# Right sides of a block-triangular solve, moved between its steps, and work for the next pair moved into an MLP stage

## The reference

```python
y[t] = r[t] @ state
Sa = state @ a[t]
state = state * w[t][None, :] - outer(Sa, b[t]) + outer(v[t], k[t])
```

## Time and profile before

| | us |
|---|---|
| median of 3 runs | 1704.86 |
| all runs | 1708.75, 1697.19, 1704.86 |
| the profiled execution | 1699.7 |
| its span in the profile | 1697.9 |
| mean granted clock of TensorE over it | 0.943 |

### The profile page before, as it was taken

One profiled execution on the slowest core, in us unless ns is written; L12 is line 12 of the kernel. 1 busy time (PEld: TensorE's weight loads), 2 busy tenths in 40 slices (PEclk: granted clock), 3 DMA queues, 4 the chain that ended last, 5 costly groups with the idle time before them and its releaser, 6 DMA issues. The chain is left out here.

```text
span 1697.9 us, 37853 instructions
## 1 busy us (share of the span) xinstructions
PE 1495.4 (88%) x15888; PEld 1296.8 (76%) x15888; DVE 801.4 (47%) x1395; ACT 423.2 (25%) x859; POOL 375.8 (22%) x314
## 2 busy tenths in 40 slices
PE   1298476998998998998996779999999999999998
PEld 0266355976876887797786769999999999999998
DVE  6866844956855765493311143333333333333332
ACT  0032233333333333333332221111111111111111
POOL 4121354323323333131232350202020201010000
PEclk9988677999998997999998989999999999999999
DMA  6534475056046126203001041000001010100011
GB/s 186 145 102 130 121 198 155 5 150 176 17 112 184 47 54 166 74 1 108 19 1 35 20 159 34 15 19 7 27 0 34 0 34 0 34 0 0 0 46 46
DMA packets 89410, 112.83 MB, mean 66 GB/s; under 512 B 10952, under 2 KB 67400, under 8 KB 89288
## 3 DMA queue, kind: packets, MB, share of 16 engines
q1 hardware_dynamic: 89288, 111.05, 23.3%
HBM read 78.73 MB, written 32.28 MB: 65 GB/s over the span
## 5 line engine op out<-in xcount | busy, mean ns | idle before, releaser
L1332 PE MATMUL banks<-x2t,u 128*128 x1536 | 377.3, 393 | 9.2 <-POOL u L1299 9.2
L1342 PE MATMUL banks<-u,hid 128*128 128x320 f32 x2304 | 360.6, 309 | 0.0
L1342 PEld LDWEIGHTS banks<-u,hid 128*128 128x128 f32 x2304 | 349.0, 188 | 11.2
L1332 PEld LDWEIGHTS banks<-x2t,u 128*128 128x128 f32 x1536 | 284.0, 189 | 62.2 <-issue 9.5
L1397 DVE SCALAR_TENSOR_TENSOR hid<-banks,hid 128x512 fp32r<-128x512 f32 x192 | 132.8, 692 | 414.5 <-ACT hid L1367 414.5
L1367 ACT ACTIVATE hid<-banks 128x512 fp32r<-128x512 f32 x192 | 115.0, 599 | 582.0 <-PE banks L1332 582.0
L769 PE MATMUL banks<-xt,wi 128*128 128x512 f32 x768 | 197.2, 400 | 19.6 <-issue 12.4
L778 PE MATMUL banks<-wo,hid 128*128 128x320 f32 x1152 | 183.8, 309 | 5.7 <-POOL hid L1169 5.7
L778 PEld LDWEIGHTS banks<-wo,hid 128*128 128x128 f32 x1152 | 175.3, 188 | 14.1 <-POOL hid L1169 6.4
L769 PEld LDWEIGHTS banks<-xt,wi 128*128 128x128 f32 x768 | 142.5, 191 | 47.5 <-issue 20.8
L1169 POOL TENSOR_TENSOR hid<-gap,hid 128x512 fp32r<-128x512 f32 x96 | 123.7, 1288 | 225.3 <-ACT hid L909 225.0
(11 more groups left out here) (105 smaller groups left out, 1558.3 us busy)
## 6 DMA issues: line engine op xcount, KB each, us to landing
scaled_operands<-made SPq DMA_DIRECT2D x42, 416.8 KB
made<-kbaw SPq DMA_DIRECT2D x42, 312.0 KB
kb<-scaled_operands SPq DMA_DIRECT2D x24, 416.0 KB
raw<-w SPq DMA_DIRECT2D x8, 640.0 KB, 5.7
lam<-scaled_operands SPq DMA_DIRECT2D x24, 209.6 KB
at<-scaled_operands SPq DMA_DIRECT2D x24, 208.0 KB
raw<-w SPq DMA_DIRECT2D x8, 512.0 KB, 4.0
rt<-rvt SPq DMA_DIRECT2D x96, 40.0 KB
```

The source lines that it names most:

```text
L1332: mm = pe.matmul(p_up[f][:], u1[:, par, w, f * 128:(f + 1) * 128], xt[:, x, cols], start=(i == 0), stop=(i == 7))
L1342: mm = pe.matmul(p_dn[t][:, 0:D], hid[:, f, h, t * 128:(t + 1) * 128], u2[:, par, w, f, :], start=(f == 0 and i == 0), stop=(f == NFU - 1 ...
```

## The change

`right_sides` takes a block b and makes only that. Block 0 stays at the head of the pair; blocks 1 to 3 go in front of the rest of their own step (block 1 in front of `turn_state`), each behind a wait for VectorE's copy of the block before. `sma_full` is raised for block 0 by the right sides, as before by all of them. `scores_low` comes ahead of `turn_answers` on PE, and their copies change places on ScalarE.

`load_kb_a` is split. `load_a` now stands in front of `load_v`, behind the decays, and waits for all four blocks of the pair's own right sides.

For the pair behind an MLP, SyncE issues the loads of v (natural), kb, r, the decays and the raw units, and the late store, in the MLP, ahead of its wait for the stage's output. The two diagonals that PE made in that pair (24 and 25, 32 and 33, 40 and 41) are made in the MLP behind the fourth `up`, into the bank of the turned answers, and ScalarE copies them in front of the output. A wait in `turn_state` keeps that bank until they are copied.

```diff
--- before.py
+++ after.py
@@ -223,17 +223,26 @@
         result_bank = pairs[3][:, 1, :]
         STATE = slice(C, C + 2 * GH // 2 * HD)
 
-        def diagonal_bank(i):
-
-            return result_bank if i < FIRST and i % 2 else state_bank
+        def drained(p):
+
+            return p % PPC == PPC - 1 and p >= PPC
+
+        def in_mlp(p):
+
+            return prepared_in(p) if p >= 0 and drained(p) else []
+
+        late_diagonals = [i for p in range(NP) for i in in_mlp(p)]
+
+        def diagonal_of(i):
+
+            if i in late_diagonals:
+                k = late_diagonals.index(i) % 2
+                return turn_bank[:, k * C:(k + 1) * C]
+            return (result_bank if i < FIRST and i % 2 else state_bank)[:, 0:C]
 
         def answer_rows(j, b):
 
             return block_of((b + 2 * j) % NB)
-
-        def drained(p):
-
-            return p % PPC == PPC - 1 and p >= PPC
 
         down_bank = [pairs[1][:, 0, :], pairs[1][:, 1, :], answer_bank, state_bank]
 
@@ -339,7 +348,7 @@
                     sp.wait_ge(op_stored[slot(i)], 16 * uses(i))
                 return scratch[2 * p:2 * p + 2, :, :].rearrange("j p w -> p j w")
 
-            def load_kb_a(p):
+            def load_kb(p):
 
                 both = both_units(p)
                 if p >= 2:
@@ -347,9 +356,13 @@
                     sp.wait_ge(low_full, p - 1)
                 sp.dma_start(kb[:, p % 2, :, :, :, :].rearrange("p j a q t -> p j (a q t)"), both[:, :, 0:OP_A])\
                     .then_inc(kb_in[p % 2], 16)
+
+            def load_a(p):
+
+                both = both_units(p)
                 if p >= 2:
                     for j in range(2):
-                        sp.wait_ge(sma_full[j], NB * (p - 2) + 1)
+                        sp.wait_ge(sma_full[j], NB * (p - 1))
                 a = at[:, p % 2, :, :, :].rearrange("p j q t -> p j (q t)")
                 sp.dma_start(a, both[:, :, OP_A:OP_LAM]).then_inc(at_in[p % 2], 16)
 
@@ -436,11 +449,13 @@
                 for i in range(FIRST):
                     store_operands(i)
                     if i == 2:
-                        load_kb_a(0)
+                        load_kb(0)
+                        load_a(0)
                         load_decays(0)
                     if i == 5:
                         load_r(1)
-                        load_kb_a(1)
+                        load_kb(1)
+                        load_a(1)
                     if 0 < i <= 8:
                         load_raw(i - 1 + RING)
 
@@ -449,34 +464,42 @@
                 for i in prepared_in(p)[1:]:
                     store_operands(i)
 
+            def early_loads(p):
+
+                if p + 1 < NP:
+                    load_v_natural(p + 1)
+                if p + 2 < NP:
+                    load_kb(p + 2)
+                if p:
+                    store_late(p - 1)
+
             def pair(p):
                 c = p // PPC
+                after_mlp = p > 0 and drained(p - 1)
                 raws = loaded_in(p)
                 if p == 0:
                     load_v(1)
-                if p + 1 < NP:
-                    load_v_natural(p + 1)
-                if p + 2 < NP:
-                    load_kb_a(p + 2)
-                if p and not drained(p - 1):
-                    store_late(p - 1)
-                for i in raws[:1]:
-                    load_raw(i)
-                if p + 2 < NP:
-                    load_r(p + 2)
-                for i in raws[1:]:
-                    load_raw(i)
+                if not after_mlp:
+                    early_loads(p)
+                    for i in raws[:1]:
+                        load_raw(i)
+                    if p + 2 < NP:
+                        load_r(p + 2)
+                    for i in raws[1:]:
+                        load_raw(i)
                 if p == 2 * PPC - 1:
                     load_tokens(0)
                 elif p % PPC == 0 and p >= 2 * PPC:
                     load_tokens(c - 1)
                 for i in prepared_in(p)[:1]:
                     store_operands(i)
-                if p and not drained(p - 1):
-                    store_tokens(p - 1)
-                if p + 1 < NP:
-                    load_decays(p + 1)
+                if not after_mlp:
+                    if p:
+                        store_tokens(p - 1)
+                    if p + 1 < NP:
+                        load_decays(p + 1)
                 if p + 2 < NP:
+                    load_a(p + 2)
                     load_v(p + 2)
                 if 0 <= p - PIECES_FROM < PIECES // 2:
                     raw_piece(2 * (p - PIECES_FROM))
@@ -486,8 +509,17 @@
                 if c < 0:
                     return
                 if last is not None:
-                    store_late(last)
+                    p = last + 1
+                    if p < NP:
+                        early_loads(p)
+                        if p + 2 < NP:
+                            load_r(p + 2)
                     store_tokens(last)
+                    if p < NP:
+                        if p + 1 < NP:
+                            load_decays(p + 1)
+                        for i in loaded_in(p):
+                            load_raw(i)
                 if c == NCH - 1:
                     load_tokens(c)
                 sp.wait_ge(x2_saved_v, 2 * (c + 1))
@@ -504,9 +536,11 @@
             def diagonal(i):
 
                 _, b_made, a_made, _ = parts(i)
-                o = diagonal_bank(i)
+                o = diagonal_of(i)
                 pe.wait_ge(scaled, 2 * (i + 1))
-                if i >= FIRST:
+                if i in late_diagonals:
+                    pe.wait_ge(ut_saved, (i - FIRST) // 2 + 1)
+                elif i >= FIRST:
                     pe.wait_ge(lt_saved, i)
                 elif i >= 2:
                     pe.wait_ge(lt_saved, i - 1)
@@ -516,25 +550,29 @@
                                        a_made[rows(s), q, block_of(b)], start=True, stop=True)
                 mm.then_inc(lt_full, 1)
 
-            def right_sides(p, j):
+            def right_sides(p, j, b):
 
                 g = 2 * (p % PPC) + j
                 o = solve_bank(j)
-                if j == 0:
-                    if p >= PPC:
-                        pe.wait_ge(state_ready, p - PPC + 1)
-                    pe.wait_ge(vn_in[p % 2], 16 * (p // 2 + 1))
-                    if p % PPC == 0 and p >= 2 * PPC:
-                        pe.wait_ge(up_saved, NF1 * (p // PPC - 1))
-                pe.wait_ge(sc_saved[j], p + 1)
-                for b in range(NB):
-                    t, d = block_of(b), slice(b * HD, (b + 1) * HD)
-                    for h, q, s in heads:
-                        pe.matmul(o[block_of(h), d], at[:, p % 2, j, q, t], st[:, g, q, rows(s)], start=b == 0, stop=False)
-                    for h, q, s in heads:
-                        mm = pe.matmul(o[block_of(h), d], nvmak[:, j, s, 1, q, t], vnat[:, p % 2, j, h, :],
-                                       start=False, stop=b == NB - 1)
-                mm.then_inc(sma_full[j], 1)
+                if b == 0:
+                    if j == 0:
+                        if p >= PPC:
+                            pe.wait_ge(state_ready, p - PPC + 1)
+                        pe.wait_ge(vn_in[p % 2], 16 * (p // 2 + 1))
+                        if p % PPC == 0 and p >= 2 * PPC:
+                            pe.wait_ge(up_saved, NF1 * (p // PPC - 1))
+                    pe.wait_ge(sc_saved[j], p + 1)
+                else:
+                    pe.wait_ge(rhs_saved[j], NB * p + b)
+                t, d = block_of(b), slice(b * HD, (b + 1) * HD)
+                for h, q, s in heads:
+                    pe.matmul(o[block_of(h), d], at[:, p % 2, j, q, t], st[:, g, q, rows(s)], start=b == 0, stop=False,
+                              skip_group_check=b > 0)
+                for h, q, s in heads:
+                    mm = pe.matmul(o[block_of(h), d], nvmak[:, j, s, 1, q, t], vnat[:, p % 2, j, h, :],
+                                   start=False, stop=True, skip_group_check=b > 0)
+                if b == 0:
+                    mm.then_inc(sma_full[j], 1)
 
             def right_side_rest(p, j, b):
 
@@ -561,6 +599,8 @@
 
                 if p:
                     pe.wait_ge(ut_saved, p)
+                    if in_mlp(p - 1):
+                        pe.wait_ge(lt_saved, diagonals_before(p + 1))
                 else:
                     pe.wait_ge(kbn_saved[1], 1)
                 for j in range(2):
@@ -708,11 +748,11 @@
                     diagonal(i)
 
             def pair(p):
-                prepared = prepared_in(p - 1)
                 after_mlp = p > 0 and drained(p - 1)
+                prepared = [] if after_mlp else prepared_in(p - 1)
                 more = p + 1 < NP
-                right_sides(p, 0)
-                right_sides(p, 1)
+                right_sides(p, 0, 0)
+                right_sides(p, 1, 0)
                 if after_mlp:
```

(21 more changed lines are left out.)

## The result

| | before | changed |
|---|---|---|
| median of 13 runs, us | 1704.06 | 1684.22 |
| lowest and highest | 1690.78, 1713.89 | 1675.84, 1695.09 |
| profiled execution and its span | 1699.7, 1697.9 | 1691.96, 1690.3 |

A forecast was written before the change was run, and what follows sets the result against it. It took PE's work plus 0.86 us of idle time per pair to bound the recurrence, with stalls and half clock lengthening some pairs. Terms summed to +1.6 us; between 1699.7 and the 1704.9 median bases it stated 1704, range 1683 to 1727.

The forecast's parts named there:

- the sum: All forecast terms over the recurrence and the pairs behind an MLP added up: +1.6 us on an execution of 1699.7.
- rival A: Heads of pairs: thinner heads remove three quarters of stalls and half-clock time, -20 in place of -2, 1686 us; chance 0.25.
- The undisturbed pair: Steady pair's head: blocks add 1.01 us, earlier scores of answers save 0.45, net +0.56; idle 0.2 then 1.2 us.
- The pairs behind an MLP: Pairs 8, 12, 16, 20: head and blocks +3.1 us; loads made in the MLP -6.7, between 0 and -10.
- Rival C: Behind an MLP: output and tokens cause the low clock, so moved loads gain 5.4 us less; 1709 us; chance 0.15.
- The load of a: Moved behind the decays: no cost there; leaving the burst at the head cuts stalls by 2 us, between 0 and -10.
- Rival B: Heads of pairs: new idle time lowers the clock, ten more falls in twelve heads, +21 us, 1725 us; chance 0.18.
- my test: Recurrence, 504 to 834 us: the prediction is wrong if the mean clock there moves by more than 0.05.

The follow-up runs named there:

- e1: Kernel before plus only the MLP part: loads and diagonals of the pair behind an MLP made in the MLP; 1688.6 us, ratio 0.9927.
- e3: Kernel before with only the load of a moved to its new place, in front of `load_v`; 1700.0 us, ratio 1.0000.
- e4: Changed kernel with all four blocks of right sides at the head again; 1685.4 us, ratio 0.9921 to before.
- e6: Changed kernel with one block at the head and the other three in one run behind the first answers; 1705.8 us, ratio 1.0028 to before.
- e11: The changed kernel measured again, unaltered, on the same chip as three other runs; 1687.4 us, ratio 0.9892 to before.
- e9: Changed kernel with block 0 of the right sides made twice at the head to fill idle time, output unchanged; 1682.6 us, ratio 0.9858 to before.
- e7: e4 with most rows of kb, a, r, v and v natural not loaded from pair 10's operands on, output wrong; 1666.4 us, ratio 0.9781 to before.
- e5: Changed kernel with the second block of right sides moved to the head too, two between the steps; 1663.1 us, ratio 0.9759 to before.

## Why the prediction came out as it did

The forecast of no measurable change, 1704 with 1683 to 1727, holds by its range and only just: 1684.2 is at its lower edge, and the sum of +1.6 us stands against some -16. That is luck of the range, which was drawn wide enough for rival A; the sum missed. The two profiles say where: pairs 0 to 7 came out at +4.4 us (the sum's terms for them give +4.3), the stages of pairs 8, 12, 16 and 20 at -8.7 (-3.6), and the other pairs at -4.7 (+2.9); the terms that are left, -2.0, were tied to no pair.

**The undisturbed pair: right.** L687, the former L647, starts 2.58 us behind the turned answers where it started 3.48 behind; the low scores are ahead of them now. The pair is 0.46 us longer (forecast 0.56), the idle time 1.28 us (1.4) and ended by the copy that was named. VectorE's update of the state splits it, 0.24 and 0.81, which I had not seen. A block costs 0.32 (from 513.46 to 513.78 in PE's timeline, forecast 0.34), and the MLPs with two diagonals in them are 1.0 us longer (61.36 to 62.4, forecast 0.9).

**The pairs behind an MLP: right in kind, mis-sized.** Stages 8, 12 and 16 are 9.4 us shorter together, pair 20's 0.7 longer as forecast (+0.7). With +0.8 for each of the three, the loads give -11.8 where my term was -6.7, "between 0 and -10". The clock did what was forecast, the pairs take 13.5, 13.2 and 13.7 us, and VectorE's wait of 5.34 us for a raw unit in pair 12 is gone. The reason for taking two thirds, output and tokens together at the head, had no effect: all four pairs run at 1.00. Alone the part gave 12 us (e1). Rival C is out.

**The load of a: no cost shows, as said; of the -2 nothing shows either** (e3: 0.0 us, give or take 5, with 15.5 us of late time ahead of diagonals, where it was 15.3).

**The term that the sum lacked: late instructions.** I read them as the effect of a burst of transfers, and let the spread of the right sides count for nothing there. e4 against the changed kernel shows that it removes 12 of 20 us, as much as the seven waits behind fast blocks cost before (11.7), and e6 that they come back with the run. It offsets most of the 0.9 us a pair that spreading costs. And the clock often falls with these waits: behind pair 8 of the kernel before, seven of the nine falls to the low level come within a wait with no releaser or up to 1.3 us behind it, and the other two are behind MLPs. This is rival A's result in part, through a cause that I gave only as "thins out all three". Three quarters of the stalls and of the low clock were to vanish; it was 61% of late time (20.1 to 7.8), and in pairs 9 to 23 half clock went from 61 to 44 us, or 34 in e11.

**Rival B came in part.** The new idle time took the clock in pairs 21 to 23 (+7.5 us in that profile, +2.5 in e11) and in pair 17, but not in the ten of twelve that would have made the change a loss. The rule of the Trainium skill that stands beside B (TensorE: Matmul & The Clock Gate, "A second HAM failure mode: psum-queue depth-cycling") agrees with e9 and with the 12 falls at 1.55 us; for the changed kernel as a whole the falls it foretells were too few to make a loss.

The mean clock from 504 to 834 us, my test, moved from 0.92 to 0.94, less than 0.05; it hides that the stages of pairs 14 to 19 all rose and pairs 22 and 23 fell.

## What to carry to other kernels

Work that can be put off is best placed where an engine would wait anyway, no more of it and no less: the head had 1.3 us of waiting, one block at it left a gap that cost clock, four made a run that outpaced its own instructions, and two or three were some 20 us better than either. A long run of very short matmuls has a price that no duration in the profile shows. Where an engine waits without a releaser, count at which instruction that is, and look whether a packet of the instruction queue has just landed, before blaming the other transfers. And loads that a queue holds back behind one wait for a stage's end can be issued inside that stage: here that was worth 12 to 20 us.

## What the runs showed of the hardware

PE waits for its own instructions at the end of some blocks of 256, which are 126.7 matmul records here. In the kernel before that cost 20.1 us, 0.2 to 2.7 us each, at 15 of 85 block ends; the longest in any kernel was 4.4 us (e4). PE went on 1.1 to 1.7 us after the end of a packet of 16,384 bytes on queue q8 in 131 of 134 cases. Either of two things is enough. One is a block run through in 1.5 to 1.7 us (seven waits before, 11.7 us). The other is a packet that starts late, by 2.6 to 4.1 us in the changed kernel, where no block was shorter than 3.9 us. With the queues at 68 GB/s in place of 96 (e7 against e4) the waits behind pair 9 fell from 14 to 6 us.

In a stretch with the same work (pairs 9 to 23 of e5 and of the changed kernel), the clock and the late instructions make most of 25 us of 450. A single idle time of 1.55 us at the head of pairs 21 to 23 went with a fall of the clock in 12 of 12 cases in four kernels, 1.24 us in 3 of 9, 0.93 us in 2 of 3, 0.63 us in none of 12. Behind 1.28 us in all per head, of which 0.8 in one piece, it fell in pair 17 of the changed kernel, and not in 9, 10, 13 and 19.
